# One signal for each head's masked scores, and one wait for each head's exponential, in the steady part of an attention and two-MLP kernel

## Chip, cores and metric

The kernel runs on one core of one Trainium2 chip. The metric is the device time of one execution, in microseconds (us). Before the change it is 1192.25 us, the median of 3 runs (1191.92 to 1192.62).

## What is computed

Chunked attention (4 batches, 8 heads, 768 positions, head size 64, with 8 memory keys and values per head), and then two MLPs on its 3072 tokens of 512 numbers. All in fp32.

```python
for c in range(nc):                      # chunks of 32 queries, keys from 16 before to 8 after
    k_full = concat(mem_k, k_ctx); v_full = concat(mem_v, v_ctx)
    scores = scale * q_c @ k_full^T
    a = exp(scores - max(scores))
    out[c] = (a / (sum(a) + 1e-9)) @ v_full
x = moe2(moe(out))                       # moe: h = relu(x @ w_in); (s*h*h + b) @ w_out
                                         # moe2: h = x @ w_in; (h * sigmoid(1.702 h)) @ w_out
```

## The kernel before

**Work and order.** Every fp32 product is made of three fast products of high and low parts (high·high, high·low, low·high), so ScalarE (ACT) makes each high part, a rounded copy, and VectorE (DVE) or GpSimd (POOL) the low part, the difference. There is no scheduler: each engine has a stream of its own, written out by hand, and waits on semaphores that count up.

A *unit* of the attention is a pair of heads on 96 queries; there are 128. The first 16 are done in a batch phase (functions whose names begin with `first_`), up to about 36 us. The other 112, the *steady units*, are woven into the first MLP of the first five token tiles (three of 384 tokens, two of 480), one *beat* for each unit, up to about 490 us. In each of an MLP's 16 steps there are 24 places, one for each matmul, and the table `AT` says before which of them PE does a piece of attention. All after about 500 us is the rest of the first MLP and the second; no line of the change runs there.

**A beat on each engine** has two groups, with n the unit whose turn it is, and LEAD = 4:

- PE (TensorE), kind 1: `transpose_probs(n+1)` (L862), `transpose_qk(n+4)` (L838, L839). Kind 2: `attend(n)` (L875), `score(n+3)` (L851).
- ACT, kind 1: `exp(n+2)` (L1101, two heads), `split_qk_hi(n+4)` (L1088), `split_pT_hi(n+1)` (L1096). Kind 2: `copy_x_hi(n)` (L1122 or L1127), and in the first tile `normalize(n+2)` (L1108).
- DVE, kind 1: `invert(n+2)` (L1446, L1450), `split_qk_lo(n+4)` (L1430), `split_pT_lo(n+1)` (L1454). Kind 2: `mask_and_max(n+3)` (L1439, two heads), `split_x_lo(n)` (L1460 or L1465). Its groups come 6 or 4 places later than PE's (`AFTER`).
- POOL: `normalize(n+2)` (L712) from the second tile on, and once in four beats `split_v` (L705, L707). In the first tile it also splits the MLP's weights (L653, L655, L660), as they are loaded.

Between these stand the MLP's own: `nonlinear` (ACT L1149, waits for PE's first product), `gate` (DVE L1490), `split_g_hi` (ACT L1157), `split_g_lo` (DVE L1496), PE's products L908 and L935, and at each tile's third step the copies of the last tile's result (ACT L1277). In the first tile ACT also rounds weights (L1166).

**The functions around the change.** `mask_and_max(n)` waits for `scored`, and for each of two heads adds the mask to the scores in PSUM, writes them to `probs` and their negated maximum to one column of `exp_bias`. L1439 is this in the profile: an operation on 96 x 128 numbers, and a read of the accumulator that writes the column. `exp(n)` on ACT takes the scores and the column of one head at a time. Before the change it waits once, for `max_ready`, which DVE raises after the second head. PE also waits for `max_ready`: `score(n)` for that of unit n-1 (the scores' bank is free again), `attend(n)` for that of unit n+2.

**A wait chain to keep in mind.** `transpose_probs(n)` on PE waits for `probs_ready` (the normalized exponentials), for `pT_ready` of the unit before (DVE's L1454, so that the bank of transposed probabilities is free) and for `qk_ready` of unit n+2. And `split_qk_lo` on DVE waits for `pT_hi_done`, which ACT's L1096 raises.

The batch phase has the same pair of functions, `first_mask_and_max` (L1399) and `first_exp` (L1075). There each head has its own signal and its own wait already:

```python
out=s_probs[i % 2][:, h, :], in0=s_bank_s[p][e][0:QT, 0:P], ...
accum_out=s_bias[:, i % 2, h:h + 1]).then_inc(s_max_ready, 1)        # L1399, each head
...
act.wait_ge(s_max_ready, 4 * i + h + 1)                              # before L1075, each head
```

Of the kernel before, what the change touches and what calls it, by code (L numbers as in the profile page):

```python
# [7 lines left out]
ALU = mybir.AluOpType  # L8
# [14 lines left out]
LEAD = 4  # L23

AFTER = {1: 6, 2: 4}
MASKED = -3.0e38
# [97 lines left out]
def there(n):  # L124
    return FIRST <= n < UNITS
# [7 lines left out]
def nth(n):  # L133

    return n - FIRST + 1
# [10 lines left out]
def bass_chunked_attention_two_ffn(nc, q, k, v, mem_k, mem_v, w_in1, w_out1, s, b, w_in2, w_out2, x2_dram, out):  # L146
    B, H, S, D = q.shape
    DM, FF = w_in1.shape
    SCALE = 1.0 / float(D) ** 0.5
# [5 lines left out]
    with ctx:  # L155
# [3 lines left out]
        def sem(name):  # L159
            return ctx.enter_context(nc.semaphore(name))  # L160
# [17 lines left out]
        exp_bias, total, inv_total, total_e = small[:, 0], small[:, 1], small[:, 2], small[:, 3, 0]  # L178
# [177 lines left out]
        max_ready = sem("max_ready")  # L356
# [88 lines left out]
        def mask_of(i):  # L445
            j = ORDER[i]
            return 0 if j % QPB == 0 else 2 if j % QPB == QPB - 1 else 1
# [319 lines left out]
        def _(pe):  # L767
# [73 lines left out]
            def score(n):  # L841
                pe.wait_ge(qk_ready, nth(n))
                if n == FIRST:
                    pe.wait_ge(zeros_ready, 1)
                    pe.wait_ge(s_max_ready, 4 * HALVES)
                if there(n - 1):
                    pe.wait_ge(max_ready, nth(n - 1))
                if there(n - LEAD):
                    pe.wait_ge(x_ready, nth(n - LEAD))
                for i, (a, c) in enumerate(((qk_hi, qk_hi), (qk_hi, qk_lo), (qk_lo, qk_hi))):  # L850
                    last = nc.tensor.matmul(bank_s[0:QT, :], a[:, n % 2, 0:QT], c[:, n % 2, QT:QT + 2 * P],  # L851
                                            start=(i == 0), stop=(i == 2))
                last.then_inc(scored, 1)
# [11 lines left out]
            def attend(n):  # L865
                j, hp = n // HP, n % HP
                if there(n - 1):
                    pe.wait_ge(x_ready, nth(n - 1))
                if there(n + LEAD - 2):
                    pe.wait_ge(max_ready, nth(n + LEAD - 2))  # L870
                if hp == 0:
                    pe.wait_ge(v_ready, j - FIRST // HP + 1)
                pe.wait_ge(pT_ready, nth(n))
                for i, (a, c) in enumerate(((v_hi, pT_hi), (v_hi, pT_lo), (v_lo, pT_hi))):
                    last = nc.tensor.matmul(bank_o, a[:, j % 2, hp * P:(hp + 1) * P], c[:, n % 2, :],  # L875
                                            start=(i == 0), stop=(i == 2))
                last.then_inc(attended, 1)

            def group(kind, n):
                if kind == 1:  # L880
                    if there(n + 1):
                        transpose_probs(n + 1)
                    if there(n + LEAD):
                        transpose_qk(n + LEAD)
                else:
                    if there(n):
                        attend(n)
                    if there(n + LEAD - 1):
                        score(n + LEAD - 1)
# [115 lines left out]
            transpose_qk(FIRST + 1)  # L1005
            first_product(0, 1, range(0, 2))
            score(FIRST)
            first_product(0, 0, range(2, KT))
            transpose_qk(FIRST + 2)
            first_product(0, 1, range(2, KT))  # L1010
            score(FIRST + 1)

            for mm in range(M0):
# [34 lines left out]
        def _(act):  # L1048
# [47 lines left out]
                nc.scalar.activation(pT_hi[:, n % 2, :], bank_pT, ACT.Copy).then_inc(pT_hi_done, 1)  # L1096

            def exp(n):
                act.wait_ge(max_ready, nth(n))
                for h in range(2):  # L1100
                    nc.scalar.activation(probs[:, n % 2, h, :], probs[:, n % 2, h, :], ACT.Exp, scale=-1.0,  # L1101
                                         bias=exp_bias[:, n % 2, h:h + 1], accum_out=total[:, n % 2, h:h + 1]
                                         ).then_inc(exp_done, 1)
# [27 lines left out]
            def group(kind, n):  # L1131
                if kind == 1:

                    if there(n + 2) and there(n):
                        exp(n + 2)
                    if there(n + LEAD) and there(n):
                        split_qk_hi(n + LEAD)
                    if there(n + 1):
                        split_pT_hi(n + 1)
                else:  # L1140
                    if there(n):
                        copy_x_hi(n)
                    if there(n + 2) and not pool_normalizes(n + 2):
                        normalize(n + 2)
# [154 lines left out]
            first_x_hi(HALVES - 1)  # L1299
            split_qk_hi(FIRST + 1)  # L1300
            exp(FIRST)
            nonlinear(0, 0)
            split_qk_hi(FIRST + 2)
# [3 lines left out]
            nonlinear(0, 1)  # L1307
            split_w_out_hi(2)
            exp(FIRST + 1)
            split_qk_hi(FIRST + LEAD - 1)  # L1310
            act.wait_ge(table_loaded, 1)
# [57 lines left out]
        def _(dve):  # L1369
            nc.vector.memset(masks[:, :, :], MASKED).then_inc(masks_filled, 1)  # L1370
            dve.wait_ge(masks_filled, 1)
            for m, shift in enumerate((-LEFT, 0, RIGHT)):
                for c in range(QT // CHUNK):
# [4 lines left out]
                    last = nc.vector.memset(masks[chunk, m, NMEM + lo:NMEM + hi], 0.0)  # L1378
            last.then_inc(masks_ready, 1)

            for buffer in (qk_hi, qk_lo):
                for h in range(2):
                    other = slice((1 - h) * D, (2 - h) * D)
                    last = nc.vector.memset(buffer[other, :, QT + h * P:QT + (h + 1) * P].bitcast(F32), 0.0)
# [49 lines left out]
            def mask_and_max(n):  # L1434
                dve.wait_ge(scored, nth(n))
                if there(n - LEAD + 1):
                    dve.wait_ge(x_hi_done, nth(n - LEAD + 1))
                for h in range(2):
                    last = nc.vector.tensor_tensor_reduce(  # L1439
                        out=probs[:, n % 2, h, :], in0=bank_s[0:QT, h * P:(h + 1) * P], in1=masks[:, mask_of(n // HP), :],  # L1440
                        scale=-SCALE, scalar=-MASKED, op0=ALU.add, op1=ALU.min, accum_out=exp_bias[:, n % 2, h:h + 1])
                last.then_inc(max_ready, 1)

            def invert(n):
                dve.wait_ge(exp_done, 2 * nth(n))
# [24 lines left out]
            def group(kind, n):  # L1470
                if kind == 1:

                    if there(n + 2) and there(n):
                        invert(n + 2)
                    if there(n + LEAD) and there(n):
                        split_qk_lo(n + LEAD)
                    if there(n + 1):
                        split_pT_lo(n + 1)
                else:
                    if there(n + LEAD - 1):  # L1480
                        mask_and_max(n + LEAD - 1)
                    if there(n):
                        split_x_lo(n)
# [151 lines left out]
            first_x_lo(HALVES - 1)  # L1635
            split_qk_lo(FIRST + 1)
            mask_and_max(FIRST)
            invert(FIRST)
            dve.wait_ge(sb_loaded, 32)
            gate(0, 0)  # L1640
            split_qk_lo(FIRST + 2)
            mask_and_max(FIRST + 1)
            split_g_lo(0, 0)
            gate(0, 1)
# [94 lines left out]
```

## Time and profile before

| | |
|---|---|
| median of 3 runs | 1192.25 us (1191.92 to 1192.62) |
| profiled execution, its own time | 1191.04 us |
| its span, first to last instruction | 1189.2 us |
| busy: PE | 1170.7 us (98%) |
| busy: DVE, ACT, POOL | 895.9 (75%), 698.6 (59%), 401.2 us (34%) |
| granted TensorE clock | 1.00 |
| chain that ended last, by engine | PE 85%, ACT 6%, DVE 4%, issue 3%, POOL 1% |

The rows name an engine, a line of the kernel, an operation and "out<-in" by the program's names (`arena_raw` holds `probs`, `small` holds `exp_bias`). PEld is TensorE's weight load, which runs beside its matmuls. "[x <-E L]" is idle time of the engine before the row, and what ended it. The profile models the ends of matmuls: one of 384 columns lasts 0.34 us in it, while the next starts 0.175 us after it.

### The profile page before, as it was taken

The numbers are of one execution on the slowest core, as the hardware profiler recorded it, in microseconds if no ns is written. First come the engines' busy times: TensorE is split into PE (matmuls) and PEld (weight loads), VectorE is DVE, ScalarE is ACT, GpSimd is POOL, SyncE is SP. The second block draws the span as 40 slices with busy tenths as digits, with TensorE's granted clock in tenths as the row PEclk, the third lists the DMA queues.
The fourth block names the chain that finished last, engine by engine and source line by source line (L and its number), as shares of the span: only waits on it lengthen the run. The fifth ranks groups of instructions, "written<-read, shape, count | busy, mean of one in ns | idle before, by whom it ended". The sixth has DMA issues, their size and how long they took to land.

```text
span 1189.2 us, 19643 instructions
## 1 busy us (share of the span) xinstructions
PE 1170.7 (98%) x6170; PEld 1010.4 (85%) x6170; DVE 895.9 (75%) x2261; ACT 698.6 (59%) x1907; POOL 401.2 (34%) x412
## 2 busy tenths in 40 slices
PE   8999999999999999999999999999999999999998
PEld 5899999999888888888888888888888888888887
DVE  7787777777777777667888957889577888577663
ACT  7788767767776776444445744446444456444452
POOL 3865222222222222323563124640245521244200
PEclk9999999999999999999999999999999999999999
DMA  7753322313132232113422424224234224222231
GB/s 149 170 136 87 66 52 52 76 43 64 35 76 63 56 89 60 37 36 104 142 71 79 146 91 142 71 72 142 71 107 142 71 80 150 89 71 71 71 115 62
DMA packets 167691, 104.28 MB, mean 88 GB/s; under 512 B 99495, under 2 KB 144039, under 8 KB 167591
## 3 DMA queue, kind: packets, MB, share of 16 engines
q1 hardware_dynamic: 166368, 102.82, 31.4%
q8 instruction: 51, 0.84, 0.3%
q14 instruction: 49, 0.40, 0.1%
q10 hardware_dynamic: 1223, 0.23, 0.1%
HBM read 89.26 MB, written 13.76 MB: 87 GB/s over the span
## 4 chain that ended last, share of the span: by engine, by line
PE 85%; ACT 6%; DVE 4%; issue 3%; POOL 1%; DVEq 0%; ACTq 0%; POOLq 0%
PE psum L976 25%; PE psum L933 22%; PE psum L935 18%; PE psum L908 11%; PE psum L851 2%; PE psum L875 2%; DVE arena L1430 2%; ACT arena_raw L1101 2%; PE psum L862 2%; ACT arena L1088 2%; ACT arena L1096 1%; PE psum L839 1%; DVE arena L1454 1%; PE psum L838 1%; PE psum L773 1%
## 5 line engine op out<-in xcount | busy, mean ns | idle before, releaser
L976 PE MATMUL psum<-weights 128*128 128x512 f32 (+1 forms) x1344 | 337.6, 386 | 0.0
L976 PEld LDWEIGHTS psum<-weights 128*128 128x128 f32 x1344 | 252.2, 188 | 49.2
L935 PE MATMUL psum<-g_hi,weights 128*128 128x384 f32 (+1 forms) x768 | 223.2, 362 | 0.0
L908 PE MATMUL psum<-arena,weights 128*128 128x384 f32 (+1 forms) x960 | 215.9, 360 | 0.2 <-DVE ffn L1490 0.2
L908 PEld LDWEIGHTS psum<-arena,weights 128*128 128x128 f32 x960 | 166.4, 188 | 9.1 <-DVE ffn L1490 0.4
L1533 DVE TENSOR_TENSOR arena_raw<-psum,arena_raw 128x512 f32<-128x512 f32 (+1 forms) x160 | 109.0, 681 | 85.5 <-PE psum L976 83.8
L712 POOL TENSOR_TENSOR arena_raw<-arena_raw,small 96x256 f32<-96x256 f32 x96 | 58.6, 610 | 271.7 <-DVE small L1450 261.3
L935 PEld LDWEIGHTS psum<-g_hi,weights 128*128 128x128 f32 x768 | 139.5, 188 | 8.8
L935 PE MATMUL psum<-g_lo,weights 128*128 128x384 f32 (+1 forms) x384 | 138.1, 360 | 0.0
L1430 DVE TENSOR_TENSOR arena<-psum,arena 128x96 fp32r<-128x96 f32 x336 | 83.2, 275 | 68.3 <-ACT arena L1096 65.9
L1101 ACT ACTIVATE arena_raw<-arena_raw,small 96x128 f32<-96x128 f32 x224 | 88.0, 394 | 78.0 <-DVE small L1439 77.6
L672 POOL TENSOR_TENSOR arena_raw<-arena_raw 128x256 f32<-128x256 f32 x32 | 28.3, 884 | 305.6 <-DMA arena_raw<-in_moe_w_in_dram 188.5
L933 PE MATMUL psum<-weights,g_hi 128*128 128x512 f32 x384 | 118.2, 389 | 0.0
L1219 ACT ACTIVATE arena_raw<-arena_raw 128x512 f32<-128x512 f32 x48 | 30.4, 633 | 129.1 <-DVE arena_raw L1533 129.1
L665 POOL TENSOR_TENSOR weights<-arena_raw,weights 128x512 fp32r<-128x512 f32 x48 | 68.6, 1442 | 85.3 <-ACT weights L1178 85.1
L933 PEld LDWEIGHTS psum<-weights,g_hi 128*128 128x128 f32 x384 | 72.1, 188 | 15.0
L1503 DVE TENSOR_TENSOR weights<-arena_raw,weights 128x1024 fp32r<-128x1024 f32 x64 | 84.4, 1320 | 0.0
L1178 ACT ACTIVATE weights<-arena_raw 128x512 fp32r<-128x512 f32 x96 | 58.5, 626 | 39.2 <-PE psum L933 26.7
L935 PEld LDWEIGHTS psum<-g_lo,weights 128*128 128x128 f32 x384 | 72.2, 188 | 5.4
L1088 ACT ACTIVATE arena<-psum 128x96 fp32r<-128x96 f32 x336 | 74.7, 256 | 2.3
L933 PE MATMUL psum<-weights,g_lo 128*128 128x512 f32 x192 | 74.7, 389 | 0.0
L933 PE MATMUL psum<-weights,arena 128*128 128x512 f32 x288 | 74.5, 389 | 0.0
(132 smaller groups left out, 2201.1 us busy)
## 6 DMA issues: line engine op xcount, KB each, us to landing
arena_raw<-in_moe_w_out_dram SPq DMA_DIRECT2D x128, 256.0 KB, 4.0
arena_raw<-in_moe_w_in_dram SPq DMA_DIRECT2D x64, 256.0 KB, 3.0
arena_raw<-in_k_dram SPq DMA_DIRECT2D x31, 240.0 KB
arena_raw<-in_v_dram SPq DMA_DIRECT2D x30, 240.0 KB
arena_raw<-x_scratch SPq DMA_DIRECT2D x3, 2048.0 KB, 10.0
arena_raw<-in_q_dram SPq DMA_DIRECT2D x31, 192.0 KB
out_dram<-result SPq DMA_DIRECT2D x5, 1024.0 KB, 5.1
result<-in_moe_w_in_dram SPq DMA_DIRECT2D x16, 256.0 KB, 3.8
```

The source lines that it names most:

```text
L665: nc.gpsimd.tensor_tensor(lo, w_out_raw(k), hi.bitcast(F32), ALU.subtract).then_inc(w_out2_now_ready, 1)
L712: nc.gpsimd.tensor_tensor(probs[:, n % 2, :, :], probs[:, n % 2, :, :], inv_total[:, n % 2, :].unsqueeze(2).to_broadcast([QT, 2, P]), ALU.mult
L908: last = nc.tensor.matmul(dst, w[:, kt * P:(kt + 1) * P], x, start=(kt + i == 0), stop=(kt == KT - 1 and i == 2))
L933: last = nc.tensor.matmul(acc[c][:, :], g[:, piece], w, start=start, stop=stop)
L935: last = nc.tensor.matmul(acc[c][:, 0:n], w[:, piece], g, start=start, stop=stop)
L976: last = nc.tensor.matmul(bank_of[bank][:, 0:width(i)], w[:, k * P:(k + 1) * P], x[:, k, :], start=(k + t == 0), stop=(k == 1 and t == 2))
L1088: last = nc.scalar.activation(qk_hi[parts, n % 2, cols], bank_qk[parts, source], ACT.Copy)
L1101: nc.scalar.activation(probs[:, n % 2, h, :], probs[:, n % 2, h, :], ACT.Exp, scale=-1.0, bias=exp_bias[:, n % 2, h:h + 1], accum_out=tota ...
L1178: nc.scalar.activation(hi, w_out_raw(k), ACT.Copy).then_inc(w_out2_hi_done, 1)
L1430: last = nc.vector.tensor_tensor(qk_lo[parts, n % 2, cols], bank_qk[parts, source], qk_hi[parts, n % 2, cols].bitcast(F32), ALU.subtract)
L1503: last = nc.vector.tensor_tensor(rows_parts(q, 1)[:, these], rows_raw[:, these], rows_parts(q, 0)[:, these].bitcast(F32), ALU.subtract)
L1533: return nc.vector.tensor_tensor(to[:, 0:w], bank_of[bank][:, 0:w], other[:, 0:w], ALU.add)
```

## The change

VectorE raises `max_ready` after each of the two heads, so its count is twice as high. PE, which needs both heads, waits for twice the number. ScalarE waits before each head's exponential for that head's own count: `2*nth(n) - 1` for head 0, `2*nth(n)` for head 1. Nothing is moved on any engine, and nothing else is changed.

```diff
@@ score(n), PE @@
-                    pe.wait_ge(max_ready, nth(n - 1))
+                    pe.wait_ge(max_ready, 2 * nth(n - 1))
@@ attend(n), PE @@
-                    pe.wait_ge(max_ready, nth(n + LEAD - 2))
+                    pe.wait_ge(max_ready, 2 * nth(n + LEAD - 2))
@@ exp(n), ACT @@
-                act.wait_ge(max_ready, nth(n))
                 for h in range(2):
+                    act.wait_ge(max_ready, 2 * nth(n) - 1 + h)
                     nc.scalar.activation(probs[:, n % 2, h, :], probs[:, n % 2, h, :], ACT.Exp, scale=-1.0,
@@ mask_and_max(n), DVE @@
                 for h in range(2):
-                    last = nc.vector.tensor_tensor_reduce(
+                    nc.vector.tensor_tensor_reduce(
                         out=probs[:, n % 2, h, :], in0=bank_s[0:QT, h * P:(h + 1) * P], in1=masks[:, mask_of(n // HP), :],
-                        scale=-SCALE, scalar=-MASKED, op0=ALU.add, op1=ALU.min, accum_out=exp_bias[:, n % 2, h:h + 1])
-                last.then_inc(max_ready, 1)
+                        scale=-SCALE, scalar=-MASKED, op0=ALU.add, op1=ALU.min, accum_out=exp_bias[:, n % 2, h:h + 1]
+                        ).then_inc(max_ready, 1)
```

## Rows read from the trace of the kernel before

**Rows 1.** Busy by stretch: us, PE PEld DVE ACT POOL (count), PEclk, DMA, GB/s

```profile
116.00:316.00 200.00, 197.53 (x1302) 187.72 (x1302) 151.51 (x657) 144.41 (x559) 52.59 (x74) 1.00 0.27 59
316.00:450.00 134.00, 129.49 (x767) 110.83 (x766) 99.58 (x440) 94.15 (x369) 37.80 (x53) 1.00 0.27 65
```

**Rows 2.** Waits, whole span: engine, line <- releaser: us in total, times, longest

```profile
ACT arena_raw L1101 <- DVE small L1439: 77.6, 75, 1.7
...
PEld psum L862 <- issue: 23.4, 52, 1.5
```

**Rows 3.** Timeline, batch phase: start us, us, instruction [idle before <- releaser]

```profile
25.16 0.29 DVE L1399 CUSTOM_DVE_ANT_0 arena_raw<-psum,masks 96x128 f32<-96x128 f32 x1
...
25.38 0.28 DVE L1399 CUSTOM_DVE_ANT_0 arena_raw<-psum,masks 96x128 f32<-96x128 f32 x1
...
25.50 0.40 ACT L1075 ACTIVATE arena_raw<-arena_raw,ffn 96x128 f32<-96x128 f32 x1 [0.68 <-DVE ffn L1399]
```

**Rows 4.** Timeline, one beat of the second tile

```profile
203.26 0.28 DVE L1439 CUSTOM_DVE_ANT_0 arena_raw<-psum,masks 96x128 f32<-96x128 f32 x1
...
203.40 0.27 PE L839 MATMUL psum<-ident,arena_raw 128*128 128x128 f32 x1
...
203.79 0.40 ACT L1101 ACTIVATE arena_raw<-arena_raw,small 96x128 f32<-96x128 f32 x1 [1.36 <-DVE small L1439]
...
204.70 0.69 ACT L1088 ACTIVATE arena<-psum 128x96 fp32r<-128x96 f32 x3
...
205.84 0.76 DVE L1430 TENSOR_TENSOR arena<-psum,arena 128x96 fp32r<-128x96 f32 x3 [0.78 <-ACT arena L1096]
...
206.63 0.36 DVE L1454 TENSOR_TENSOR arena<-psum,arena 128x192 fp32r<-128x192 f32 x1
...
207.06 0.20 PEld L862 LDWEIGHTS psum<-ident,arena_raw 96*128 96x128 f32 x2 [0.23 <-issue]
```

**Rows 5.** Lines L862 and L1101, 116 to 316 us: idle before (us, times)

```profile
  issue: 9.0, 26
...
  DVE small L1439: 45.7, 46
```

**Rows 6.** Timeline around rows 4: POOL beside DVE, and PE behind

```profile
200.07 0.62 DVE L1496 SCALAR_TENSOR_TENSOR g_lo<-ffn,columns,g_hi 128x384 fp32r<-128x384 f32 x1
...
206.39 1.28 POOL L707 TENSOR_TENSOR arena<-arena_raw,arena 128x512 fp32r<-128x512 f32 x1
...
206.91 1.18 DVE L1496 SCALAR_TENSOR_TENSOR g_lo<-ffn,columns,g_hi 128x384 fp32r<-128x384 f32 x1
...
209.13 0.41 PEld L875 LDWEIGHTS psum<-arena 128*128 128x128 f32 x3 [0.41 <-issue]
```

**Rows 7.** Timeline: ACT's copies of a tile's result

```profile
227.62 0.87 ACT L1277 ACTIVATE result<-psum 128x384 f32<-128x384 f32 x2 [0.93 <-PE psum L935]
```

**Rows 8.** L1101, 34 to 116 us: idle before; then a beat's timeline

```profile
  DVE small L1439: 5.4, 7
...
74.00 0.40 ACT L1101 ACTIVATE arena_raw<-arena_raw,small 96x128 f32<-96x128 f32 x1 [0.74 <-DVE small L1439]
...
77.39 0.70 ACT L1108 ACTIVATE arena_raw<-arena_raw,small 96x128 f32<-96x128 f32 x2
...
78.13 0.20 PEld L862 LDWEIGHTS psum<-ident,arena_raw 96*128 96x128 f32 x2 [0.55 <-ACT arena_raw L1108]
```

**Rows 9.** Timeline, three beats of the fourth tile (480 tokens): ACT

```profile
338.86 0.57 ACT L1149 ACTIVATE ffn<-psum 128x480 f32<-128x480 f32 x1 [0.76 <-PE psum L908]
...
339.45 0.40 ACT L1101 ACTIVATE arena_raw<-arena_raw,small 96x128 f32<-96x128 f32 x1
...
354.44 0.57 ACT L1149 ACTIVATE ffn<-psum 128x480 f32<-128x480 f32 x1 [1.07 <-PE psum L908]
...
354.90 0.39 ACT L1101 ACTIVATE arena_raw<-arena_raw,small 96x128 f32<-96x128 f32 x1
...
432.17 0.40 ACT L1101 ACTIVATE arena_raw<-arena_raw,small 96x128 f32<-96x128 f32 x1
```

## The prediction

> **What bounds the kernel now.** I read the page's busy times first. PE is busy 98% of the span (1170.7 of 1189.2 us), so a change on DVE and ACT can only win what PE loses by waiting. The busy times by stretch say where that is: in 116 to 316 us PE is idle 2.5 us, in 316 to 450 us 4.5 us [rows 1]. That understates it. A matmul's modelled end runs 0.17 us past the point where the next could have started, so a stall shorter than that isn't seen as idle time at all. The weight load of the waiting instruction shows it better, and the list of waits has it: before L862, `transpose_probs`, the weight load sat idle 52 times for 23.4 us [rows 2]. Not all of it is loss. Before the load at 207.06 it shows 0.23 us [rows 4], while the matmuls around it start at 206.81 and 207.09 where 0.175 us is due: 0.11 us lost. So I take 0.12 us off each, and 23.4 us stand for about 17 us of lost PE time; in the first tile a few more waits are booked under ACT. L862 is by far the largest place where PE loses time in the steady part.
>
> The same list says that ACT sat idle before L1101, the exponential, 75 times of 112, until DVE's L1439, the mask: 77.6 us [rows 2]. That is ACT's idle time, and by itself it costs nothing. The question is whether the mask's end is on the way to L862.
>
> The timeline of a beat says that it is [rows 4]. The exponential starts at 203.79, when the mask's second head is done, L1088 at 204.70 when both exponentials are through; L1096 follows it at once and ends 0.78 us of idle time of DVE, whose L1430 starts at 205.84; then comes L1454 at 206.63, and PE's weight load for L862 at 207.06. So nothing in the 3.3 us between the exponential's start and PE's has slack. And DVE's next mask stands behind L1454 in its own queue. The loop mask, exponential, L1088, L1096, L1430, L1454, next mask runs over ACT and DVE alone, without PE. In 116 to 316 us this loop is a little slower per beat than PE's own work, and PE stops at L862 for the difference.
>
> **The change, part by part.** *The exponential of head 0 starts earlier.* The batch phase already works in the new way, with the same shapes, so its rows give the size [rows 3]. There the mask of a head starts at 25.16, the next head's at 25.38, and the exponential of the first at 25.50: 0.34 us after its mask began. In the steady beat it is 203.79 less 203.26, 0.53 us [rows 4]. The difference is 0.19 us, and the step from one head's mask to the next is 0.22 us. I take 0.21 us for each exponential that now waits for its mask. Head 1's mask ends 0.21 us after head 0's and head 1's exponential starts 0.40 us after head 0's, so its new wait is always over when it is reached, and the whole chain behind moves up by 0.21 us.
>
> *The second signal on DVE, the second wait on ACT, the doubled numbers on PE.* Zero. In rows 3 every head signals and DVE still goes from one to the next in 0.22 us. No instruction is moved past a queue, and PE waits for the same event as before. The bounds are 0 and 0.02 us for each of 112 units, 2 us; I keep 0 because the nearest rows, the same operation with the signal, show no difference.
>
> *What this is worth, by stage.*
>
> First tile, 34 to 116 us. Here seven exponentials waited for the mask, 5.4 us in all [rows 8]; in the other beats ACT was late itself and an earlier mask gives nothing. In the beat of rows 8 ACT then works without a gap from 74.00 to the end of L1108, its normalizing, at 78.09, and PE's load starts at 78.13 after 0.55 us idle. So each of the seven gives its 0.21 us: **1.5 us**.
>
> Second and third tile, 116 to 316 us. PE waited at L862 26 times, 9.0 us [rows 5]; less 0.12 each that makes 5.9 us. Twice (near 136 and 231 us) the exponential in front stood behind the copies L1277, which wait for PE themselves, 0.93 us at 227.62 [rows 7]; those two stalls, 0.28 us each, stay. That leaves 5.3 us. Four times PE also stalled at L875, `attend`, which waits for the mask too: 0.41 us of the load's idle time [rows 6], some 0.27 us of loss each, 1.1 us. So 6.4 us can be won. Against that stand 46 beats whose exponential waits for the mask [rows 5], 46 x 0.21 = 9.7 us. More than is lost, so the loop falls below PE's own time per beat, and then DVE and ACT gain a little ground on PE in each beat, which the next long stall uses up. How much ground can be kept? In the beat of rows 4 ACT's L1088, at 204.70, needs of PE only the transpose L839, which is over at 203.67, so up to 1.0 us can be. I count on most of it, but not all, since the four disturbed places need up to 0.7 us within two beats: **5.6 us**. Bounds: 3.7 us if nothing is carried from beat to beat (each stall then shrinks by at most 0.21), 6.4 us if everything is.
>
> Fourth and fifth tile, 316 to 500 us. PE idles most here [rows 1], but little of it is within reach. Every second exponential stands behind L1149, and that waits for PE's product L908 (1.07 us of idle time at 354.44). Without waiting for the mask it follows 0.46 us after L1149 (354.90); that is PE waiting for ACT waiting for PE, and the mask has no part in it. In seven such beats, the first at 339.45 and the last at 432.17, it follows after 0.59 us because the mask was later [rows 9]: 0.12 us each, **0.8 us**. The exponentials in between gain 0.21 us, and PE has slack there: nothing. One stall at the start (319.6 us) with a late mask in front gives 0.2 to 0.5, I take **0.3 us**; one near 480 us **0.2 us**.
>
> Together 1.5 + 5.6 + 0.3 + 0.8 + 0.2 = 8.4 us. The profiled execution took 1191.04 us, which makes 1182.6 us; the median of the runs is 1.2 us above that execution, so I forecast 1192.25 - 8.4 = **1183.9 us**.
>
> *What is late next.* PE itself, for most of the second and third tile. In the fourth, L1149 behind L908, which the change doesn't touch.
>
> *Where POOL and DVE meet.* In rows 6 POOL's L707 runs from 206.39 for 1.28 us, and DVE's L1496 beside it takes 1.18 us; without POOL it takes 0.62 us. The next mask and PE's L875 are late after that. The Trainium skill, in SBUF — State Buffer, section "SBUF: two separate sides", says that a DVE operation with two SBUF inputs and a GpSimd operation that reads SBUF use one pair of ports, which whoever comes first holds for its whole length. By that rule the change could cost time as well as win it, because it shifts DVE by some tenths against POOL; at its worst it would give the 1197 us of rival C instead of 1183.9. The row agrees for this operation.
>
> In my sum it costs nothing, since POOL's `split_v` stands behind its own normalizing and so moves with DVE. In the first tile POOL's weight splits follow loads, which don't move; there I allow 1 us either way for it.
>
> **Rivals.** *A: nothing is carried over.* The ground gained in one beat is lost again at some instruction that waits for PE, so each stall shrinks by 0.21 us at most. For it: L1149, L1088, L1096 and the mask all wait for PE at some place. Against it: the 1.0 us of slack above, and idle ACT (1.36 us) ahead of each exponential. Then 1.5 + 3.7 + 0.2 + 0.8 + 0.2 = 6.4 us: 1185.9 us, and 4 us (1188.3) if the first tile and the small terms fail as well.
>
> *B: the exponential starts earlier and PE gains nothing,* because L1088 or L1430 then meets another wait, or because the first head's signal reaches ACT no earlier than the second's did. For it: only that every wait has several conditions, of which the trace names one. Against it: rows 3, where this very signal works, and the chain of rows 4 without a gap. The gain is under 2.4 us: 1190 to 1192.5 us, about 1191.
>
> *C: slower.* With DVE shifted against POOL, L1496 or `invert` meets `split_v` in more beats than now. Price: 1.18 less 0.62, 0.56 us a meeting. Now 4 of the meetings stop PE; there are 28 `split_v`. If all met and each delayed PE in full, that is 24 more, 13.4 us against a gain of 8.4: 1197 us. It decides from 15 more meetings on. Against it: `split_v` hangs on DVE's own `invert` over POOL's normalizing, so they keep their distance.
>
> **How the numbers follow.** Forecast (gain over 7 us) 0.6, A 0.25, B 0.11, C 0.04. One measurement of this kernel tells 0.2%, 2.4 us, from no change. Forecast and nearly all of A are beyond that: faster 0.85; B, with the weakest end of C, is 0.12; slower 0.03. For the range I add the upper bounds: 1.5 + 6.4 + 0.5 + 0.8 + 0.4 = 9.6 us, and 1 us of luck with POOL in the first tile, 10.6: 1181.7 us. Below it reaches to A's weak end, a gain of 3.8 us: 1188.5 us. Left out are B, C and a rest, some 0.17.
>
> **What would show it.** ACT's idle time before L1101 until L1439 falls by about 0.21 us for each of 75 (from 77.6 to some 60 us, less where the loop now waits for PE). The first exponential starts 0.33 us after its mask's start instead of 0.53. The L862 loads wait in 116 to 316 us fewer than 10 times, 26 now, and the L875 stalls go. In 316 to 450 us PE's idle time falls by 1 us at most. I am wrong if L862 still waits 20 times there, or if ACT shows a new wait for PE in every beat.

## The result, and the profile after

The changed kernel takes **1182.4 us**, median of 4 runs (1182.08 to 1182.70); the kernel before took 1192.37 us beside it (4 runs, 1191.92 to 1192.62). The ratio is 0.9917, with a 95% interval of 0.9900 to 0.9934: 10 us faster, where 8.4 were forecast. The two profiled executions took 1191.04 and 1182.08 us, 8.96 us apart, and their spans differ by as much. The medians differ by 1 us more because the profiled execution of before was itself 1.3 us under its median, and that of after 0.3 us. Below I account for the 9.0 us between the traces. Whether the tenth microsecond belongs to the change isn't shown; how the first beats scatter by about as much stands at the head of the experiments.

The page of the changed kernel: span, busy times, the chain that ended last, and the group of the exponential.

```profile
span 1180.2 us, 19643 instructions
...
PE 1166.2 (99%) x6170; PEld 1012.9 (86%) x6170; DVE 895.8 (76%) x2261; ACT 700.0 (59%) x1907; POOL 401.3 (34%) x412
...
PE 90%; ACT 4%; DVE 3%; issue 2%; POOL 1%; DVEq 0%; POOLq 0%; ACTq 0%
...
L1101 ACT ACTIVATE arena_raw<-arena_raw,small 96x128 f32<-96x128 f32 x224 | 87.7, 393 | 44.7 <-DVE small L1439 44.0
```

DVE and ACT are as busy as they were. What went is PE's idle time, and PE's share of the last chain rose from 85% to 90%. Busy time of PE fell by 4.5 us as well, with the same 6170 matmuls. I read that as stalls too short to show as idle time, which the modelled ends of matmuls count as busy, as the prediction said of them.

The same stretches as [rows 1] (PE, PEld, DVE, ACT, POOL; then clock, DMA share, GB/s):

```profile
116.00:316.00 200.00, 199.15 (x1341) 194.94 (x1339) 156.45 (x680) 150.13 (x577) 55.72 (x78) 1.00 0.27 60
316.00:450.00 134.00, 130.90 (x776) 112.92 (x774) 101.05 (x441) 95.67 (x372) 36.95 (x53) 1.00 0.31 74
```

In 116 to 316 us PE's idle time fell from 2.47 to 0.85 us, and it did 39 more matmuls in the same 200 us. The granted clock is 1.00 in both kernels.

The waits over the whole span that answer to [rows 2], and two that have grown, L1149 from 24.8 us in 33 waits and L1127 from 4.1 us in 7 (engine, line <- releaser: us in total, times, longest; "issue" is a wait for which the profile names no releaser):

```profile
ACT arena_raw L1101 <- DVE small L1439: 44.0, 57, 1.5
ACT ffn L1149 <- PE psum L908: 28.0, 42, 1.7
...
ACT arena L1127 <- PE psum L851: 15.8, 37, 1.0
...
PEld psum L862 <- issue: 13.2, 23, 1.5
```

The weight load of L862, `transpose_probs`, waits 23 times instead of 52. In 116 to 316 us it is 5 times for 2.3 us, where it had been 26 times for 9.0 us [rows 5]. L862 and then L1101 in that stretch, idle before them (us, times; the row with L1454 is idle time of PE itself at one of the five, and not a sixth wait):

```profile
  issue: 2.3, 5
  DVE arena L1454: 0.6, 1
...
  DVE small L1439: 21.1, 31
```

The beat that answers to [rows 4], at the same unit:

```profile
199.97 0.28 DVE L1439 CUSTOM_DVE_ANT_0 arena_raw<-psum,masks 96x128 f32<-96x128 f32 x1
...
200.29 0.40 ACT L1101 ACTIVATE arena_raw<-arena_raw,small 96x128 f32<-96x128 f32 x1 [0.66 <-DVE small L1439]
...
200.60 0.27 PE L839 MATMUL psum<-ident,arena_raw 128*128 128x128 f32 x1
...
201.19 0.69 ACT L1088 ACTIVATE arena<-psum 128x96 fp32r<-128x96 f32 x3
...
202.34 0.76 DVE L1430 TENSOR_TENSOR arena<-psum,arena 128x96 fp32r<-128x96 f32 x3 [0.78 <-ACT arena L1096]
...
203.13 0.36 DVE L1454 TENSOR_TENSOR arena<-psum,arena 128x192 fp32r<-128x192 f32 x1
...
204.01 0.32 PEld L862 LDWEIGHTS psum<-ident,arena_raw 96*128 96x128 f32 x2
```

The exponential now starts 0.32 us after its mask's start; it was 0.53. The links behind it are as they were: L1088 0.90 us after the exponential (0.91), L1430 1.15 us after that (1.14), L1454 0.79 us after that (0.79). But L1454 ends at 203.49 and PE's load starts at 204.01, with no idle time before it: the chain is 0.52 us ahead of PE, where before PE stood waiting at its end.

### The profile page after: what moved, and what is told of

Same layout as the page of the kernel before. It is cut to its first block, busy times and chain, and to the rows that moved or that the text cites. A ratio compares the mean times of both kernels' runs of the same rounds, so it can differ in the third digit from the quotient of the medians.

```text
span 1180.2 us, 19643 instructions
## 1 busy us (share of the span) xinstructions
PE 1166.2 (99%) x6170; PEld 1012.9 (86%) x6170; DVE 895.8 (76%) x2261; ACT 700.0 (59%) x1907; POOL 401.3 (34%) x412
## 4 chain that ended last, share of the span: by engine, by line
PE 90%; ACT 4%; DVE 3%; issue 2%; POOL 1%; DVEq 0%; POOLq 0%; ACTq 0%
PE psum L976 26%; PE psum L933 22%; PE psum L935 20%; PE psum L908 13%; PE psum L851 3%; PE psum L875 2%; PE psum L862 2%; ACT arena_raw L1101 1%; DVE arena L1430 1%; PE psum L839 1%; ACT arena L1088 1%; PE psum L838 1%; PE psum L773 1%; ACT arena L1096 0%; DVE arena L1454 0%
## 5 line engine op out<-in xcount | busy, mean ns | idle before, releaser
L908 PE MATMUL psum<-arena,weights 128*128 128x384 f32 (+1 forms) x960 | 215.7, 360 | 0.0
L908 PEld LDWEIGHTS psum<-arena,weights 128*128 128x128 f32 x960 | 166.3, 188 | 8.8 <-DVE ffn L1490 0.2
L712 POOL TENSOR_TENSOR arena_raw<-arena_raw,small 96x256 f32<-96x256 f32 x96 | 58.6, 610 | 263.5 <-DVE small L1450 263.5
L1430 DVE TENSOR_TENSOR arena<-psum,arena 128x96 fp32r<-128x96 f32 x336 | 83.2, 275 | 62.6 <-ACT arena L1096 59.9
L1101 ACT ACTIVATE arena_raw<-arena_raw,small 96x128 f32<-96x128 f32 x224 | 87.7, 393 | 44.7 <-DVE small L1439 44.0
L1088 ACT ACTIVATE arena<-psum 128x96 fp32r<-128x96 f32 x336 | 74.9, 257 | 2.5
```

The lines of the kernel that those rows point to most:

```text
L712: nc.gpsimd.tensor_tensor(probs[:, n % 2, :, :], probs[:, n % 2, :, :], inv_total[:, n % 2, :].unsqueeze(2).to_broadcast([QT, 2, P]), ALU.mult
L908: last = nc.tensor.matmul(dst, w[:, kt * P:(kt + 1) * P], x, start=(kt + i == 0), stop=(kt == KT - 1 and i == 2))
L1088: last = nc.scalar.activation(qk_hi[parts, n % 2, cols], bank_qk[parts, source], ACT.Copy)
L1430: last = nc.vector.tensor_tensor(qk_lo[parts, n % 2, cols], bank_qk[parts, source], qk_hi[parts, n % 2, cols].bitcast(F32), ALU.subtract)
```

## The experiments

All comparisons below are with runs of the kernel before, made beside them; its medians there were 1192.40, 1191.82 and 1191.90 us. By **ground** I mean how much earlier than in the kernel before PE starts L862 of the k-th steady unit (k from 0 to 111), taken from the two profiled executions. Differences of ground within a stage tell what that stage won. Ground up to k = 1 scatters, from 0.2 us ahead of the kernel before to 2.6 us behind it, so I start there. About 1 us of that goes with how POOL and DVE meet. In four of the thirteen traces (the signals without the wait, every second unit, the kernel before without v's low part, and the later nonlinear operation) POOL's weight splits start ahead of DVE's L1496 near 40 and 45 us, or within 0.01 us of it. L1496 then takes 1.46 to 1.71 us and 1.45 to 1.51 us, where it is 0.61 to 0.84 us in the other nine, and the ground falls by 0.8 to 1.0 us between k = 0 and 1, against 0.2 us at most in the others.

The measured ground of the changed kernel by stage, beside the prediction's terms:

| stage | units k | forecast, us | measured, us |
|---|---|---|---|
| ahead of the first tile's second beat | to 1 | 0 | 0.23 |
| first tile | 1 to 16 | 1.5 | 0.67 |
| second and third tile | 16 to 66 | 5.6 | 6.62 |
| start of the fourth | 66 to 69 | 0.3 | 0.17 |
| fourth tile | 69 to 98 | 0.8 | 1.00 |
| up to the last unit | 98 to 111 | 0.2 | 0.28 |
| sum | | 8.4 | 8.97 |

**The signals without the wait.** DVE signals each head, PE waits for doubled numbers, ACT still waits once, for both heads. Against the kernel before:

```diff
@@ exp(n), beside the changed score, attend and mask_and_max @@
+                own = False
                 for h in range(2):
+                    if own:
+                        act.wait_ge(max_ready, 2 * nth(n) - 1 + h)
+                    elif h == 0:
+                        act.wait_ge(max_ready, 2 * nth(n))
```

> VectorE signals head by head and every waiter's number is doubled, but ScalarE still waits for both heads before its first exponential. My theory, that only the earlier start of head 0's exponential gains: no change from the kernel before, within 0.5 us (1192.4), and the first exponential starts 0.53 us after its mask as before. Rival, that the signal itself costs: up to 2 us slower.

Measured: 1192.51 us (10 runs, 1191.86 to 1192.97), ratio 1.0001 (0.9991 to 1.0011). Its list of waits is that of [rows 2] again:

```profile
ACT arena_raw L1105 <- DVE small L1443: 76.8, 74, 1.7
```

(L1105 and L1443 are L1101 and L1439; the lines are shifted by the edit.) So 112 more signals and the doubled numbers cost nothing that 10 runs can tell, at most 1.3 us by the interval, and ground from k = 1 on stays within 0.12 us in each stage. The whole gain comes from ACT's first wait ending earlier.

**Each stage by itself.** The same kernel with another condition for `own`, which says where each head has its own wait.

```diff
-                own = False
+                own = n - FIRST <= 16                        # first tile
+                own = 17 <= n - FIRST <= 66                  # second and third
+                own = 17 <= n - FIRST <= 66 and n % 2 == 0   # every second one of these
+                own = n - FIRST >= 67                        # the rest
```

First tile:

> As the changed kernel, but only the first 17 steady units (the first tile) let head 0 go alone. The trace of the changed kernel shows PE 0.90 us ahead at the 17th unit, since seven gains of 0.2 us are followed by one new stall of 0.42 us at the 8th unit. My theory: that and no more, 0.9 us gain (1191.5), with the same new stall near 73 us and the long L1496 near 64.6 us. If the new stall comes from elsewhere: 1.4 us.

Measured: 1191.03 us (8 runs, 1190.63 to 1192.01), ratio 0.9990 (0.9979 to 1.0000), 1.4 us, at the edge of what the runs can tell. Ground from k = 1 to 16: 0.65 us, as in the changed kernel (0.67), with the expected long L1496 at 65 us and the new stall behind it.

Second and third tile:

> As the changed kernel, but only the 50 units whose beats fall into the second and third tile (the 18th to the 67th steady unit) let head 0 go alone; the others wait for both heads. My theory, ground carried from beat to beat: a gain of about 6.6 us (1185.8), with the L862 stalls and the four L875 stalls in 116 to 316 us gone but for two of 0.28 us. Rival A, nothing carried: 3.7 us (1188.7).

Measured: 1185.29 us (1184.59 to 1185.86), ratio 0.9939 (0.9924 to 0.9954), 7.1 us. Ground from k = 16 to 66: 6.62 us, as in the changed kernel. Rival A, where each stall shrinks by 0.21 us at most, allowed 3.7.

Every second one of them:

> As e2_middle, but only every second of those 50 units lets head 0 go alone. Ground carried over: each of about 23 waiting exponentials takes 0.21 us from the loop over ScalarE and VectorE, whether or not PE stalls in its own beat: 4.2 to 4.9 us gain (1187.5 to 1188.2). Rival A, nothing carried: only units whose own beat has a stall count, half of 3.7: about 1.9 us gain (1190.5).

Measured: 1187.74 us (1187.23 to 1188.34), ratio 0.9960 (0.9945 to 0.9975), 4.7 us. Ground from k = 16 to 66: 4.45 us out of 25 exponentials, 0.18 us for each. That is more than half of 6.62: early exponentials in beats without a stall pay for stalls in other beats. Ground is carried from beat to beat.

The rest:

> As the changed kernel, but only the units from the 68th steady one on let head 0 go alone, those of the fourth and fifth tile. The trace of the changed kernel shows 1.45 us gained from there on: 0.14 at once, eight beats of 0.10 to 0.14 us in the fourth tile, 0.20 near 480 us. My theory: 1.3 to 1.5 us gain over the kernel before. With the first tile's 0.9 and the middle's 6.6 us this makes the whole 9.0 us of the two spans. Rival: the stages help each other, and late alone gains less than 0.7 us.

Measured: 1190.48 us (10 runs, 1189.86 to 1191.62), ratio 0.9990 (0.9981 to 1.0000), 1.4 us. By ground it is 0.22 + 0.96 + 0.25 = 1.43 us; in the table these stages have 0.17 + 1.00 + 0.28 = 1.45.

The three disjoint parts gain 1.4, 7.1 and 1.4 us by their medians, 9.9 together, and the whole 10.0. These medians are no surer than their intervals, about 1 us each way. Ground says it more sharply: each part in its own stage gives 0.65, 6.62 and 1.43 us, 8.70 together, and the changed kernel has 8.74 from k = 1 on. So the stages are independent.

**The meetings of POOL and DVE taken away,** from the kernel before and from the changed one. POOL's L707, the subtraction that makes the low part of v, becomes a write of zeros, so the low part of v is left out of the products.

```diff
-                nc.gpsimd.tensor_tensor(v_lo[:, j % 2, :], v_raw, v_hi[:, j % 2, :].bitcast(F32), ALU.subtract
-                                        ).then_inc(v_ready, 1)
+                nc.gpsimd.memset(v_lo[:, j % 2, :].bitcast(F32), 0.0).then_inc(v_ready, 1)
```

From the kernel before:

> The kernel before, with GpSimd writing zeros to v_lo in place of the subtraction L707 (the low part of V is left out of the result). So no long GpSimd operation that reads SBUF stands beside VectorE's L1496 in the second and third tile. My theory: the four L1496 of 1.18 to 1.33 us there fall to 0.62 us, and since the loop over VectorE and ScalarE has no slack in the kernel before, each meeting's delay reaches PE: 2.0 to 2.5 us gain (about 1190.1), perhaps 0.5 us more for the two meetings elsewhere. If the meetings cost PE nothing: no change.

Measured: 1188.70 us (10 runs, 1187.85 to 1190.34), ratio 0.9973 (0.9964 to 0.9983), 3.1 us. Ground from k = 16 to 66: 2.44 us. The place of [rows 6] in its timeline (all lines are one less; L1495 is L1496):

```profile
208.14 0.53 POOL L707 MEMSET arena<- 128x512 f32 x1
208.68 0.61 DVE L1495 SCALAR_TENSOR_TENSOR g_lo<-ffn,columns,g_hi 128x384 fp32r<-128x384 f32 x1
```

DVE's operation is back at 0.61 us from 1.18, and the stalls at L875 are gone. The ground rises at the four beats behind the meetings and hardly elsewhere: by 0.71, 0.57, 0.72 and 0.57 us, at k = 28, 40, 52 and 64. Over the 50 beats the four meetings cost the kernel before 2.44 us, 0.61 each: they weren't only the L875 stalls (0.27 each in the prediction) but also a part of the L862 stalls that follow.

From the changed kernel:

> The changed kernel with the same edit (GpSimd writes zeros in place of L707). My theory: there the loop is ahead of PE when a meeting comes, so taking the meetings away gains little: 0 to 0.8 us against the changed kernel's 1182.4. If the gain of the change were independent of the meetings, this would gain the same 2 to 2.5 us as the edit gives the kernel before: about 1180.

Measured: 1181.47 us (1181.17 to 1181.79), ratio 0.9913 (0.9899 to 0.9928). Against the changed kernel the ground from k = 16 to 66 is only 0.26 us. The same four meetings are there in the changed kernel, and cost it a tenth of what they cost before. The one that answers to [rows 6]:

```profile
202.88 1.30 POOL L707 TENSOR_TENSOR arena<-arena_raw,arena 128x512 fp32r<-128x512 f32 x1
...
203.41 1.19 DVE L1496 SCALAR_TENSOR_TENSOR g_lo<-ffn,columns,g_hi 128x384 fp32r<-128x384 f32 x1
...
205.79 0.47 PEld L875 LDWEIGHTS psum<-arena 128*128 128x128 f32 x3
```

DVE loses the same 0.57 us, but L875 has no idle time before it any more (0.41 us in [rows 6]). The two pairs together split the 6.62 us: with no meetings the change gains 6.62 + 0.26 - 2.44 = 4.44 us there, and the other 2.2 us are losses to the meetings that the slack now absorbs.

**The exponential last.** Can more be won by taking the exponential off the chain of [rows 4] altogether? On the changed kernel, ACT's `exp(n+2)` goes behind its copies, and DVE's `invert(n+2)` behind its differences.

```diff
@@ ACT, kind 1 (on DVE the same with invert and the low parts) @@
-                    if there(n + 2) and there(n):
-                        exp(n + 2)
                     if there(n + LEAD) and there(n):
...
                         split_pT_hi(n + 1)
+                    if there(n + 2) and there(n):
+                        exp(n + 2)
```

> The changed kernel, with the exponentials of a beat put behind split_qk_hi and split_pT_hi on ScalarE, and invert behind split_qk_lo and split_pT_lo on VectorE. The exponential is on PE's way only because L1088 and L1096 stand behind it in ScalarE's queue: with the order turned, mask and exponential leave the loop, and L1454 ends earlier. Then the stalls of 0.34 us in every second beat of the fourth tile (14 of them, 4.7 us) and others go: up to 7 us faster than the changed kernel, 1175.5 to 1180. Rival: the exponential now starts up to 1.0 us later, so normalizing becomes what PE waits for at L862, above all in the first tile where ScalarE does it: no gain or up to 5 us slower.

Measured: 1211.79 us (1211.14 to 1212.70), ratio 1.0166 (1.0149 to 1.0183), 29 us over the changed kernel. A beat of the second tile:

```profile
201.34 0.28 PE L839 MATMUL psum<-ident,arena_raw 128*128 128x128 f32 x1
...
201.65 0.69 ACT L1088 ACTIVATE arena<-psum 128x96 fp32r<-128x96 f32 x3 [0.93 <-PE psum L839]
...
202.59 0.39 ACT L1101 ACTIVATE arena_raw<-arena_raw,small 96x128 f32<-96x128 f32 x1
...
203.86 0.15 DVE L1446 TENSOR_SCALAR small<-small 96x2 f32<-96x2 f32 x1
204.05 0.16 DVE L1450 RECIPROCAL small<-small 96x2 f32<-96x2 f32 x1
...
204.29 0.61 POOL L712 TENSOR_TENSOR arena_raw<-arena_raw,small 96x256 f32<-96x256 f32 x1 [3.31 <-DVE small L1450]
...
204.95 0.20 PEld L862 LDWEIGHTS psum<-ident,arena_raw 96*128 96x128 f32 x2 [0.20 <-POOL arena_raw L712]
```

ACT idles 0.93 us for PE's L839 with the masked scores ready since about 200.9. The exponential follows at 202.59, the reciprocal waits in DVE's queue, and the normalizing on POOL ends at 204.90, 0.05 us ahead of PE's load. I conclude that the loop now runs through PE and POOL. In the changed kernel the exponential ahead of L1088 costs that copy little, because most of it fills time in which ACT would wait for PE anyway: L1088 starts 0.59 us after L839's start there (201.19 and 200.60) and 0.31 us after it here, and the 0.28 us between are less than the 0.52 us by which the chain is ahead. By ground against the changed kernel, 3.7 us are lost in the first tile, 11.2 in the second and third and 13.1 in the fourth; I have read the cause in the second tile alone.

**The nonlinear operation behind the attention's group.** In the fourth tile every second exponential stands behind L1149, which waits for PE's L908. On the changed kernel, there and in the fifth, the order of the two is turned round.

```diff
-                        if place == 12:
+                        if place == 12 and mm < 3:
                             nonlinear(mm, f)
...
+                        if place == 12 and mm >= 3:
+                            nonlinear(mm, f)
```

> The changed kernel, with nonlinear (L1149) in the fourth and fifth tile put behind the attention's group of its place on ScalarE, where it stands ahead of it now. If the 0.34 us stalls there come from exponentials that stand behind L1149, which waits for PE's L908, they go: 14 stalls, up to 4.7 us faster, 1177.7 to 1180. Rival: L1149 is then some 2 us late, gate on VectorE with it, and PE or VectorE's next mask waits for that: no change or slower.

Measured: 1200.0 us (1198.84 to 1201.03), ratio 1.0069 (1.0054 to 1.0084), 17.6 us over the changed kernel. A beat of the fourth tile (L1492, L1456 and L1441 are `gate`, L1454 and the mask):

```profile
347.49 0.56 ACT L1149 ACTIVATE ffn<-psum 128x480 f32<-128x480 f32 x1
...
348.09 0.72 DVE L1492 SCALAR_TENSOR_TENSOR ffn<-psum,columns,ffn 128x480 f32<-128x480 f32 x1 [1.85 <-ACT ffn L1149]
...
349.78 0.36 DVE L1456 TENSOR_TENSOR arena<-psum,arena 128x192 fp32r<-128x192 f32 x1
350.06 0.28 DVE L1441 CUSTOM_DVE_ANT_0 arena_raw<-psum,masks 96x128 f32<-96x128 f32 x1
...
350.37 0.20 PEld L862 LDWEIGHTS psum<-ident,arena_raw 96*128 96x128 f32 x2 [1.55 <-issue]
```

L1149 is now late, DVE stands 1.85 us in front of `gate`, and everything in DVE's queue behind it, L1454 and the next mask, is late with it. PE's load waits 1.55 us. By ground against the changed kernel the whole loss lies in the fourth tile, 17.7 us from k = 66 to 98, and the turned order costs nothing in the fifth.

**The exponential last, only where it stands behind L1149.** In the 16 beats of the fourth tile whose exponential can't start early, it is moved behind the copies as in the last but one experiment, on the changed kernel.

```diff
+BEHIND_NONLINEAR = {n for pos, made in AT.items() for kind, n in made
+                    if kind == 1 and pos // (24 * NF) == 3 and pos % 24 == 12}
...
-                    if there(n + 2) and there(n):
+                    if there(n + 2) and there(n) and n not in BEHIND_NONLINEAR:
                         exp(n + 2)
...
                         split_pT_hi(n + 1)
+                    if there(n + 2) and there(n) and n in BEHIND_NONLINEAR:
+                        exp(n + 2)
```

> The changed kernel, with the turned order of e8_exp_last (exponentials behind L1088 and L1096 on ScalarE, invert behind L1430 and L1454 on VectorE) only in the 16 beats of the fourth tile whose group stands behind nonlinear. There L1149 waits for PE, and in the changed kernel the exponential, L1088 and L1096 all follow it. Turned round, L1088 and L1096 come 0.77 us earlier, and PE's 14 stalls of 0.32 to 0.35 us are too short to matter against that; the exponential comes 0.9 us later, and POOL's normalizing would end at about the moment that PE needs it. My theory: 3 to 4.7 us faster than the changed kernel, 1177.7 to 1179.5. Rival, as in e8_exp_last, normalizing becomes the last wait: up to 5 us slower than the changed kernel.

Measured: 1185.16 us (1185.02 to 1185.28), ratio 0.9943 (0.9928 to 0.9957), 2.4 us over the changed kernel. My theory fell. First the changed kernel, then this one (L864 is L862, L714 is L712, L1458 is L1454):

```profile
349.63 0.36 DVE L1454 TENSOR_TENSOR arena<-psum,arena 128x192 fp32r<-128x192 f32 x1
...
350.21 0.20 PEld L862 LDWEIGHTS psum<-ident,arena_raw 96*128 96x128 f32 x2 [0.53 <-issue]
```

```profile
350.41 0.36 DVE L1458 TENSOR_TENSOR arena<-psum,arena 128x192 fp32r<-128x192 f32 x1
...
351.12 0.61 POOL L714 TENSOR_TENSOR arena_raw<-arena_raw,small 96x256 f32<-96x256 f32 x1 [4.66 <-DVE small L1454]
...
351.90 0.20 PEld L864 LDWEIGHTS psum<-ident,arena_raw 96*128 96x128 f32 x2 [0.70 <-issue]
```

In the changed kernel L1454 is the last thing PE waits for: in all 15 stalls of the fourth tile the load follows its end by 0.22 to 0.23 us. Here L1454's work is done at 350.77, 1.13 us ahead, but the normalizing runs until 351.73 and PE's load follows at 351.90, and in all 16 such beats it follows the normalizing's end by 0.17 to 0.18 us. The stall comes back every second beat all the same, and the period of two beats is 7.79 us (344.13, 351.90, 359.70) where the changed kernel has 7.65 (342.56, 350.21, 357.87): 0.14 us times 16 is 2.2 of the 2.4 us. The transposed copies had been made early enough; the probabilities themselves were late.

**The changed kernel again,** beside this last one:

> The changed kernel once more, beside the next two on the same chip: 1182 to 1183 us, 9 to 10 us below the kernel before.

Measured: 1182.73 us (1182.44 to 1182.89), ratio 0.9922 (0.9907 to 0.9937). None of the orders tried beats it; the one faster kernel, without the low part of v, computes less.

## Why the prediction was right, and where its sizes were not

*The path.* Right. The mask's end was on the way to L862 in the second and third tile, by the loop of [rows 4], and moving the exponential moved PE. The experiment with the signals alone excludes anything else in the change, and the 10 us themselves exclude rival B, which allowed 2.4.

*The step, 0.21 us, taken from [rows 3].* Right: 0.53 less 0.32.

*The signals at zero.* Right: ratio 1.0001, when the wait is left as it was.

*First tile, 1.5 us.* Over-sized; 0.67 measured, and 0.65 with the change there alone. The step itself came as forecast: of the seven waiting exponentials the first, at 36.22 us, starts 0.21 us earlier but lies ahead of k = 1, where the scatter covers it, and the other six give 0.19 to 0.21 us each, 1.2 us together. What is missing of those 1.2 us is one meeting of POOL and DVE. The prediction set POOL's weight splits aside with "1 us either way", and that is where it went. POOL and DVE around 65 us, first of the kernel before:

```profile
65.03 0.62 DVE L1496 SCALAR_TENSOR_TENSOR g_lo<-ffn,columns,g_hi 128x384 fp32r<-128x384 f32 x1
65.23 1.57 POOL L660 TENSOR_TENSOR weights<-result,weights 128x512 fp32r<-128x512 f32 x1 [2.36 <-ACT weights L1166]
```

and of the changed kernel:

```profile
64.58 1.29 POOL L660 TENSOR_TENSOR weights<-result,weights 128x512 fp32r<-128x512 f32 x1 [2.15 <-ACT weights L1166]
64.60 1.69 DVE L1496 SCALAR_TENSOR_TENSOR g_lo<-ffn,columns,g_hi 128x384 fp32r<-128x384 f32 x1
...
73.23 0.20 PEld L862 LDWEIGHTS psum<-ident,arena_raw 96*128 96x128 f32 x2 [0.57 <-ACT arena_raw L1108]
```

Before, DVE came first by 0.20 us, and POOL's L660 took 1.57 us instead of 1.29. Now POOL comes first by 0.02 us, and DVE's L1496 takes 1.69 us instead of 0.62. Two beats later PE waits at L862, at 73.23, and the beat that ends there takes 4.97 us where it took 4.52; the beat ahead of it lost 0.07 us too. That is so in every trace: the beat takes 4.97 us in all five where L1496 is long at 65 us (1.68 to 1.72 us), and 4.52 us in the seven others whose first tile has the old order of the streams. One of these seven is the changed kernel without v's low part, where the exponentials are early too but L660 happens to come 0.56 us after DVE's operation. So the change made one meeting, worth 0.5 us: rival C's mechanism at one place, and at L660, not at L707 as rival C had it. How L1496's delay reached L862 two beats later I haven't traced. The step that failed is "loads don't move": L660 doesn't follow a load there, it follows ACT's L1166, which moves with the change.

*Second and third tile, 5.6 us.* Under-sized by 1.0. The prediction counted the 6.4 us of loss that could be won and took most, since the ground carried might not cover four disturbed places. It did cover them: in 116 to 316 us there are four stalls left that show 0.28 to 0.41 us of idle load. Two of them, at 134.8 and 227.4 us, are those behind L1277 that the prediction left standing. A fifth, 0.88 us at 311.87, was 1.01 us at 319.53 before and thus outside that stretch. With every second exponential early 4.45 us were won, against 1.9 without carrying. The measured 6.62 lies 0.2 us over my upper bound. Where the 0.2 us come from stays open; I haven't taken it further.

*Fourth tile and later.* 0.17, 1.00 and 0.28 us for 0.3, 0.8 and 0.2. Of the 1.00 us, 0.87 came in seven beats of 0.10 to 0.14 us each, for which the prediction had seven times 0.12. L1149 behind L908 stays as it was: 346.47 with 1.07 us of idle time, and the exponential at 346.94, 0.47 us behind it. The two orders that tried to get round it both lost. PE's idle time in 316 to 450 us fell by 1.4 us and not by 1 at most; the work comes 8 us earlier now, so the stall of 1.01 us at 319.53 [before] isn't in that stretch any more.

*ACT's idle time before L1101.* Forecast some 60 us, measured 44.0. Where the loop is ahead of PE, ACT waits for PE in another place: in 116 to 316 us L1127, the copy of `attend`'s result, waited for PE 4 times for 1.8 us before and 33 times for 13.4 us now, and its twin L1122, which hadn't waited, 10 times for 4.0 us. "Less where the loop now waits for PE" named this, but my 60 left it out. It costs nothing, as PE is busy then. The prediction's last sign of being wrong, "a new wait for PE in every beat", has all but come true with these 43 waits in some 50 beats, while the forecast held. It was no sign of that: what decides is how far ahead of PE's need the wait ends.

*What is late next.* PE itself, as forecast: 0.85 us of idle time in the 200 us of the second and third tile.

*Rival A* is excluded by the ground from k = 16 to 66, 6.62 and 4.45 us against its 3.7 and 1.9. It expected that ACT would meet a wait for PE in each beat, and ACT does, at L1127. But in the beat shown the chain ends 0.52 us ahead of need all the same, so such a wait limits how much ground is carried and not whether.

*Luck.* The sum is nearer than its terms. The first tile gave 0.8 us less than forecast and the second and third 1.0 us more, and these nearly cancel in 8.4 forecast and 9.0 measured.

## What to carry to other kernels

Where a small loop over two engines is a little slower than the engine that bounds the kernel, shortening it by a fifth of a microsecond a beat can be worth more than the stalls' sum suggests one by one: once the loop is the faster one, its lead absorbs the irregular delays too (here four meetings that had cost 0.61 us each). So count what the bounding engine loses in all, and expect nearly all of it, once (beats that gain) x (gain) is well above it; here it was 9.7 us against a loss of 6.4, and 6.6 came.

A signal per part instead of one per group is worth it where the consumer takes the parts one at a time and its first wait is on the chain. Moving the consumer's work in the queue is another matter: the exponential's place costs little as long as it fills a wait for PE, and all three other orders were slower.

When an edit shifts an engine by some tenths, look for pairs of DVE and POOL operations that start within that distance of each other, and at what each of them waits for.

## What the runs showed of the hardware that I had not expected

*Who is a little later pays in full, and 0.2 us turn it round.* In the pair of rows at 65 us DVE's L1496 takes 0.62 us and POOL's L660 1.57 us when DVE starts 0.20 us ahead. DVE's takes 1.69 us and POOL's 1.29 us when POOL starts 0.02 us ahead. Each time the first runs at its own length, and the second ends after about the sum: 64.60 + 1.69 = 66.29, against 64.58 + 1.29 + 0.62 = 66.49. The Trainium skill, in SBUF — State Buffer, section "SBUF: two separate sides", calls this an exclusive lock and not a bandwidth split, held by whichever started first for the whole instruction; the rows agree within 0.2 us. Who starts first can't be told from the rows at a hundredth of a microsecond: with the exponential last behind L1149 alone, DVE's operation starts at 65.25 and POOL's at 65.26, and DVE still pays (1.72 us). With DVE 0.08 us ahead (40.09, and POOL's L655 at 40.17, in the kernel with the second and third tile alone) DVE runs its 0.61 us and POOL takes 1.68. What the rows add is the asymmetry of the price in this kernel: POOL's 0.28 us cost PE nothing, and DVE's 1.07 us cost PE 0.5.

*A write of zeros by POOL doesn't disturb.* With L707 as a MEMSET, the four long L1496 of the second and third tile are gone, and the kernel before is 3.1 us faster. The same section of the Trainium skill restricts the lock, for a DVE operation with two SBUF inputs, to GpSimd operations that read SBUF. At 208 us the two operations don't overlap (208.14 + 0.53 ends before 208.68), but at 161 us of the same trace they do:

```profile
161.37 0.53 POOL L707 MEMSET arena<- 128x512 f32 x1
...
161.78 0.61 DVE L1495 SCALAR_TENSOR_TENSOR g_lo<-ffn,columns,g_hi 128x384 fp32r<-128x384 f32 x1
```

DVE's operation starts 0.12 us ahead of the MEMSET's end. Had it been held until then it would take 0.73 us, and it takes its 0.61. It is the same at 256.14 us, and at two places of the changed kernel without v's low part, so the runs agree with it, over overlaps of 0.12 to 0.13 us.

*A second wait on ACT shows no cost.* From the first exponential's start to the second's it is 0.40 us in the beat above (200.29 to 200.69), with a wait on `max_ready` between them. In the fourth tile, where both masks are long done, it is 0.38 us (346.94 to 347.32). The 0.02 us aren't the second wait's: in the kernel before, which has none, it is 0.40 us too wherever the first exponential waited for its mask (75 beats), and 0.38 us where it didn't.
